# Linear attention by blocks of 64 tokens on quarter and half arrays, with scores and r stacked as one stationary operand

## The reference, cut to what matters

```
B, H, S, D = 4, 8, 768, 48
for t in range(S):
    cur = einsum('bhd,bhe->bhde', u * kt, vt)
    y[:, :, t] = einsum('bhd,bhde->bhe', rt, state + cur)
    state = w * state + einsum('bhd,bhe->bhde', kt, vt)
x = y as (3072, 384)
h = x @ w_in (384 x 2048);  g = max(h, 0) + alpha * min(h, 0);  x2 = g @ w_out (2048 x 384)
then 8 experts of 384 tokens each, chosen by the scores x2 @ w_gate
```

## Time and profile before

| | |
|---|---|
| median of 3 runs (lowest to highest) | 891.94 us (891.16 to 891.98) |
| the profiled execution | 890.23 us, span 888.5 us |
| PE busy | 832.6 us, 94% of the span |
| DVE, POOL, ACT busy | 461.7 us, 463.2 us, 212.3 us |
| chain that ended last | 82% of it on PE, 9% on DVE |

### The profile page before, as it was taken

The page is one execution under the profiler, slowest core; times in us unless marked ns, Lnnn a source line. Parts: engine busy times, 40 slices in busy tenths (PEclk is TensorE's granted clock), DMA queues, the critical chain, the costliest instruction groups (busy, mean ns, idle before and its releaser), DMA issues.

```text
span 888.5 us, 14960 instructions
## 1 busy us (share of the span) xinstructions
PE 832.6 (94%) x5562; PEld 723.7 (81%) x5562; DVE 461.7 (52%) x1005; ACT 212.3 (24%) x440; POOL 463.2 (52%) x448
## 2 busy tenths in 40 slices
PE   3989999999999999999999999955999999999996
PEld 2978887888788878887888888745888989989996
DVE  8554546444544464446444433367766767755221
ACT  1023312111211121112111221103142443333451
POOL 5669845443544444444444253206347757667872
PEclk9999999999999999999999999955999999999999
DMA  8454411111111111111000000014405405325410
GB/s 220 125 149 132 120 51 34 54 54 54 53 53 53 53 53 53 53 53 53 9 9 9 10 10 18 10 37 170 169 23 175 171 26 196 131 67 197 180 41 27
DMA packets 42788, 70.12 MB, mean 79 GB/s; under 512 B 5489, under 2 KB 28145, under 8 KB 42737
## 3 DMA queue, kind: packets, MB, share of 16 engines
q1 hardware_dynamic: 35632, 53.71, 18.6%
q0 software_dynamic: 3072, 9.44, 3.2%
q10 hardware_dynamic: 4032, 6.29, 2.5%
HBM read 59.99 MB, written 9.44 MB: 78 GB/s over the span
## 4 chain that ended last, share of the span: by engine, by line
PE 82%; DVE 9%; issue 4%; POOL 2%; ACT 1%; DMA 1%; POOLq 0%; SPq 0%; ACTq 0%; DVEq 0%
PE bank L981 22%; PE bank L983 20%; PE bank L982 20%; PE bank L1014 5%; PE bank L993 3%; PE bank L1025 3%; PE bank L1136 3%; PE bank L1010 2%; PE bank L1074 2%; DVE grid L879 1%; DVE grid L881 1%; PE bank L1037 1%; PE bank L1162 1%; PE bank L1152 1%; DVE xTl L667 1%
## 5 line engine op out<-in xcount | busy, mean ns | idle before, releaser
L384 POOL TENSOR_TENSOR gl<-g,gh 128x512 fp32r<-128x512 f32 x96 | 124.3, 1295 | 213.1 <-ACT gh L501 213.1
L716 DVE TENSOR_SCALAR q<-bank,alpha_sb 128x512 f32<-128x512 f32 x96 | 72.1, 751 | 173.8 <-PE bank L983 173.4
L501 ACT CAST gh<-g 128x512 fp32r<-128x512 f32 x96 | 59.6, 621 | 406.0 <-PE bank L983 363.0
L981 PE MATMUL bank<-gh,wout_h 128*128 128x512 f32 x288 | 120.3, 418 | 0.7 <-POOL gl L384 0.2
L981 PE MATMUL bank<-xTh,win_h 128*128 128x512 f32 x288 | 114.5, 398 | 5.6 <-DVE xTl L667 4.4
L983 PE MATMUL bank<-gh,wout_l 128*128 128x512 f32 x288 | 113.1, 393 | 0.0
L983 PE MATMUL bank<-xTh,win_l 128*128 128x512 f32 x288 | 112.7, 391 | 0.0
L982 PE MATMUL bank<-xTl,win_h 128*128 128x512 f32 x288 | 112.7, 391 | 0.0
L982 PE MATMUL bank<-gl,wout_h 128*128 128x512 f32 x288 | 112.4, 390 | 0.0
L436 POOL TENSOR_TENSOR w1l<-raw,w1h 128x384 fp32r<-128x384 f32 x64 | 66.3, 1036 | 60.3 <-ACT w2h L534 60.0
L981 PEld LDWEIGHTS bank<-xTh,win_h 128*128 128x128 f32 x288 | 54.4, 189 | 19.2 <-issue 6.1
(11 more groups left out here) (163 smaller groups left out, 1550.5 us busy)
## 6 DMA issues: line engine op xcount, KB each, us to landing
raw<-w SPq DMA_DIRECT2D x32, 768.0 KB, 5.7
kt<-kT SPq DMA_DIRECT2D x48, 96.0 KB, 2.5
rt<-rT SPq DMA_DIRECT2D x48, 96.0 KB, 2.6
kn<-kN SPq DMA_DIRECT2D x24, 192.0 KB, 2.8
rn<-rN SPq DMA_DIRECT2D x24, 192.0 KB, 2.9
vn<-v SPq DMA_DIRECT2D x24, 192.0 KB, 3.2
x2rows<-x2n SPq DMA_DIRECT2D x24, 192.0 KB, 1.9
x2T<-w_in ACTq DMA_DIRECT2D x12, 256.0 KB, 3.5
```

What stands on the lines that cost most here:

```text
L384: nc.gpsimd.tensor_tensor(gl[:, f % 2], g[:, f % 2], gh[:, f % 2].bitcast(F32), ALU.subtract).then_inc(gl_ready, 1)
L501: nc.scalar.copy(gh[:, f % 2], g[:, f % 2]).then_inc(gh_ready, 1)
L716: nc.vector.tensor_scalar(q[:, f % 2], h, 0.0, alpha_sb[:, f:f + 1], ALU.min, ALU.mult).then_inc(q_ready, 1)
L981: nc.tensor.matmul(o, a_h, b_h, start=first, stop=False)
```

## The change

A block keeps its 128 tokens, but is computed as two halves of 64 (j = 0, 1). For each half one stationary operand (`both`) holds the masked scores of 64 tokens in one half of the partitions and scaled r in the other, and one streamed operand (`vs`) holds the 64 rows of v and the state of 48 rows. `attend` is then 16 products of 128 rows and 64 stationary columns (in the first stage j = 0 has no state and takes 64 rows), `scores` 16 of 48 rows and 64 columns, `new_state` 16 of 64 rows and 48 columns. There are two states for each block, so `update` and `decay` come twice; `update` of half 0 now stands ahead of `attend`, and `new_state` ahead of `attend`. `scale` takes three instructions, k and r live in two buffers that are loaded after the scores two blocks before, v is loaded twice, and the loop over chunks is written out. In the first stage the order on PE and DVE is a new one. The diff, cut to its core (`attend`, `update` and the loops of before stand above):

```diff
+        def halves(j):
+            return slice(j * HALF, j * HALF + HALF)
+        def heads_in(j):
+            return slice((1 - j) * HALF, (1 - j) * HALF + D)
+        def y_bank(c):
+            return banks[0] if first(c) else banks[7]
+        def score_bank(c, b, j):
+            return banks[1 + j] if first(c) and b % 2 else banks[5 + j]
+        def state_bank(c, j):
+            return banks[3 + j] if first(c) else banks[5 + j]
+        def weights(c, b):
+            if not first(c) or b == 0:
+                return both
+            return (g[:], xT[:, 0:2], q[:])[b - 1].rearrange("p d (h t) -> p d h t", h=H)
...
             def load_rows(c, b):
-                for dst, src in ((kn, kN), (rn, rN), (vn, v)):
+                for dst, src in ((kn, kN), (rn, rN)):
                     sp.dma_start(dst[:, b], src[bass.ds(c, 1), :, b].rearrange("a t d -> (a t) d")).then_inc(rows_loaded[b], 16)
+                for j in range(2):
+                    sp.dma_start(vs[halves(j), b, j], v[bass.ds(c, 1), halves(j), b].rearrange("a t d -> (a t) d")).then_inc(v_loaded[b], 16)
+                sp.dma_start(vn[:, b], v[bass.ds(c, 1), :, b].rearrange("a t d -> (a t) d")).then_inc(v_loaded[b], 16)
 
...
+            def load_next_heads(c, b):
+                wait(sp, scores_done, 8 * c + 2 * b + 2)
+                sp.sem_inc(load_begun, 1)
+                if b + 2 < B:
+                    load_heads(c, b + 2)
+                else:
+                    load_heads(c + 1, b - 2)
...
             def decay(c, b):
 
-                pool.wait_ge(y_done, B * c + b + 1)
-                nc.gpsimd.tensor_tensor(state[:, b], state[:, b], cpow[:], ALU.mult).then_inc(s_decayed, 1)
+                pool.wait_ge(v_loaded[b], 48 * c + 48)
+                wait(pool, s_updated, 8 * c + 2 * b)
+                nc.gpsimd.tensor_tensor(decayed[:].rearrange("p (h d) -> p h d", h=H), vs[:, b, 0].rearrange("p (h d) -> p h d", h=H), cpow[:], ALU.mult).then_inc(s_decayed, 1)
+            def decay2(c, b):
+                pool.wait_ge(s_updated, 8 * c + 2 * b + 1)
+                nc.gpsimd.tensor_tensor(decayed[:].rearrange("p (h d) -> p h d", h=H), vs[:, b, 1].rearrange("p (h d) -> p h d", h=H), cpow[:], ALU.mult).then_inc(s_decayed2, 1)
...
                         if f % 4 == 0:
+                            decay(i + 1, b)
                             own(i + 1, b)
-                        if f % 4 == 1:
-                            decay(i + 1, b)
-                        if f % 4 == 2 and b + 1 < B:
-                            prepare(i + 1, b + 1)
+                        if f % 4 == 2:
+                            decay2(i + 1, b)
+                            if b + 1 < B:
+                                prepare(i + 1, b + 1)
...
+            pool.wait_ge(tables, 1)
+            prepare(0, 0)
             for b in range(B):
-                prepare(0, b)
+                if b + 1 < B:
+                    prepare(0, b + 1)
...
             def scale(c, b):
                 dve.wait_ge(heads_loaded[b], 64 * c + 64)
-                nc.vector.tensor_tensor(rt[:, b], rt[:, b], rpow[:], ALU.mult).then_inc(rk_scaled, 1)
-                nc.vector.tensor_tensor(kt[:, b], kt[:, b], kpow[:], ALU.mult).then_inc(rk_scaled, 1)
+                if not first(c):
+                    dve.wait_ge(y_done, B * c + b)
+                nc.vector.tensor_tensor(kt[:, b % 2], kt[:, b % 2], kpow[:], ALU.mult).then_inc(rk_scaled, 1)
+                for j in range(2):
+                    rows = halves(1 - j)
+                    nc.vector.tensor_tensor(weights(c, b)[rows, j], rt[rows, b % 2], rpow[rows], ALU.mult).then_inc(rk_scaled, 1)
 
...
             def mask(c, b):
...
+                for j in range(2):
+                    dve.wait_ge(scores_done, 8 * c + 2 * b + j + 1)
+                    rows = halves(j)
+                    nc.vector.tensor_tensor(weights(c, b)[rows, j], score_bank(c, b, j)[rows].rearrange("p (h t) -> p h t", h=H),
+                                            before[rows, rows].unsqueeze(1).to_broadcast([HALF, H, HT]), ALU.mult).then_inc(masked, 1)
 
...
+            def update(c, b, j):
+                to, of = heads_in(1 - j), heads_in(j)
+                if j == 0:
+                    dve.wait_ge(state_done, B * c + b + 1)
+                    if not first(c):
+                        dve.wait_ge(s_decayed, B * (c - 1) + b + 1)
+                    ins = nc.vector.tensor_copy(vs[to, b, 1], state_bank(c, j)[of, 0:DM]) if first(c) else nc.vector.tensor_tensor(
+                        vs[to, b, 1], state_bank(c, j)[of, 0:DM], decayed[of], ALU.add)
+                    ins.then_inc(s_updated, 1)
                     if first(c):
-                        ins = nc.vector.tensor_copy(state[rows, b, :, cols], new[rows, :, cols])
...
+                        nc.vector.tensor_tensor(decayed[to].rearrange("p (h d) -> p h d", h=H), state_bank(c, j)[of, 0:DM].rearrange("p (h d) -> p h d", h=H),
+                                                cpow[of], ALU.mult).then_inc(s_decayed2, 1)
+                else:
+                    if not first(c):
+                        dve.wait_ge(y_done, B * c + b + 1)
+                    dve.wait_ge(s_decayed2, B * c + b + 1)
+                    nc.vector.tensor_tensor(vs[to, b, 0], state_bank(c, j)[of, 0:DM], decayed[of], ALU.add).then_inc(s_updated, 1)
...
                         if f % 4 == 1:
+                            update(i + 1, b, 0)
+                        if f % 4 == 2:
                             attended(i + 1, b)
-                        if f % 4 == 2:
-                            update(i + 1, b)
-                        if f % 4 == 3 and b + 1 < B:
-                            scale(i + 1, b + 1)
-                            own(i + 1, b + 1)
+                        if f % 4 == 3:
+                            update(i + 1, b, 1)
+                            if b + 1 < B:
+                                scale(i + 1, b + 1)
+                                own(i + 1, b + 1)
...
             def scores(c, b):
-                pe.wait_ge(rk_scaled, 8 * c + 2 * b + 2)
-                wait(pe, masked, 8 * c + 2 * b - (2 if first(c) else 0))
+                pe.wait_ge(rk_scaled, 12 * c + 3 * b + 3)
+                if first(c):
+                    wait(pe, masked, 2 * b - 2)
+                else:
+                    pe.wait_ge(s_updated, 8 * c + 2 * b)
                 wait(pe, x2n_ready, B * (c - 2) + b + OUT_PRE)
                 wait(pe, logits_ready, B * (c - 2) + b + OUT_PRE)
...
+                for h in range(H):
+                    for j in range(2):
+                        mm = nc.tensor.matmul(score_bank(c, b, j)[halves(j), h * HT:(h + 1) * HT], kt[heads_in(j), b % 2, h], weights(c, b)[heads_in(j), j, h],
+                                              start=(h == 0), stop=(h == H - 1), skip_group_check=True)
+                        if h == H - 1:
                             mm.then_inc(scores_done, 1)
 
...
             def new_state(c, b):
+                pe.wait_ge(v_loaded[b], 48 * c + 48)
+                pe.wait_ge(kpad_ready, B * c + b + 1)
                 if first(c):
                     wait(pe, s_updated, 2 * b)
                 else:
-                    pe.wait_ge(x_ready, B * c + b + 1)
-                pe.wait_ge(kpad_ready, B * c + b + 1)
...
+                for h in range(H):
+                    cols = slice(h * D, (h + 1) * D)
+                    for j in range(2):
+                        mm = nc.tensor.matmul(state_bank(c, j)[heads_in(j), cols], kpad[halves(j), b % 2, cols], vs[halves(j), b, j, cols],
+                                              start=(h == 0), stop=(h == H - 1), skip_group_check=True)
                 mm.then_inc(state_done, 1)
+            def attend(c, b):
+                pe.wait_ge(s_updated, 8 * c + 2 * b + 1)
+                pe.wait_ge(masked, 8 * c + 2 * b + 2)
+                if first(c):
+                    wait(pe, x_ready, b)
+                elif isinstance(c, int) and c == 1 and b == 0:
+                    pe.wait_ge(first_l, B)
+                else:
+                    pe.wait_ge(xt_ready, B * (c - 1) + b)
+                for h in range(H):
+                    cols = slice(h * D, (h + 1) * D)
+                    for j in range(2):
+                        rows = halves(0) if first(c) and j == 0 else slice(0, P)
+                        mm = nc.tensor.matmul(y_bank(c)[halves(j), cols], weights(c, b)[rows, j, h], vs[rows, b, j, cols],
+                                              start=(h == 0), stop=(h == H - 1), skip_group_check=True)
+                mm.then_inc(y_done, 1)
...
-                        (scores, attend, new_state, turn)[f % 4](i + 1, f // 4)
+                        (scores, new_state, attend, turn)[f % 4](i + 1, f // 4)
...
-            for n in range(NPAIR):
-                mm = nc.tensor.transpose(banks[7][:, n * P:(n + 1) * P], down[:, n], ident)
```

(60 more changed lines are left out.)

140 lines of the change are left out of this document (49 added, 91 removed).

## The result

The changed kernel takes 907.4 us (median of 4 runs, 902.5 to 909.3) beside 891.95 for the kernel before: ratio 1.0167, with an interval from 1.0126 to 1.0208. It is 1.7% slower, where I had forecast 888 us. The profiled execution took 909.3, its span is 907.6 us.

The account below looks back on a forecast made before the run. PE was taken to bound the dense layer, busy 22.35 of 22.35 us per block. 890.2 - 24.0 + 14.2 + 3.5 + 2.0 = 885.9; the median lies 1.7 higher: 888 us, own range 880 to 896, overall 869 to 908.

Parts of the forecast that it names:

- attention parts shorter, 20 blocks: Dense layer: `scores`, `new_state` and `attend` together fall from 4.88 to 3.68 us per block, -24.0 us for 20.
- DVE late at steady block ends: Dense layer outside chunk 0: scalings end at 184.1, `scores` could start at 184.65; nothing late, so no cost.
- block ends of chunk 0, waits: POOL's weight work stretches DVE's scalings; PE waits 1.6, about the same and 0.3 us, +3.5 us.
- chunk starts: The third scaling ends about 0.4 us after `scores` had started before; five chunk starts, +2.0 us.
- first stage: Four blocks: `attend` +2.8 and `new_state` unchanged per block, plus 3 us for the new chain; +14.2 us.
- column halves run side by side: Dense-layer `attend`: members sharing rows but differing in columns run at once, 0.058 us a pair, 1.27 us in all.
- The alternation of 64 and 128 rows in the first stage: `attend` changes division at each of 16 products, 0.39 us each, so 6.2 us per block.
- its reading against the change: First stage: divisions differing in rows alone count as two modes and drain the array; +14.2 us, otherwise -2.2.
- The load of 64 columns: Dense-layer attention on the divided array: half of 0.107 plus the same 0.005, so 0.058 us.
- The step that failed: DVE at dense-layer block ends: `update` 0.50 us, then three scalings 0.60 apart; nothing late, by 0.5 us.
- rival 3: DVE late at every block end as POOL's `gl` doubles the last scaling; 0.7 us x 12, 896 us, chance 0.09.
- Rival 1: Column halves load one after the other; `attend` 1.79 + 0.34 us in the dense layer; 907 us, chance 0.30.

Follow-up runs that it names:

- e1: Changed kernel with the next block's three scalings one quarter of a block earlier; 898.1 us, ratio 0.9963 to the kernel before.
- e8: Changed kernel with one added wait: POOL's `gl` in a block's last quarter starts only after DVE's three scalings; 888.5 us, ratio 0.9962 to the kernel before.
- e5: e1 with dense-layer `attend` issuing all products of column half 0, then all of half 1; 900.9 us, ratio 1.0112 to the kernel before.
- e9: e4 with 64 rows for half 0 in dense-layer `attend`, alternating with 128, result altered; 936.8 us, ratio 1.0527 to the kernel before.
- e4: Changed kernel with the edits of e1 and e3, and a chunk's first scalings ahead of the preceding chunk's end; 871.2 us, ratio 0.9771 to the kernel before.
- e2: Changed kernel with first-stage `attend` issuing its eight 64-row products first, then its eight 128-row ones; 905.3 us, ratio 1.0028 to the kernel before.
- e3: Changed kernel with 128 rows in all first-stage `attend` products, half 0's update moved behind `attend`; 906.0 us, ratio 1.0051 to the kernel before.
- e7: Changed kernel without any edit, run on another chip; 906.5 us, ratio 1.0166 to the kernel before.

## Why the prediction was wrong

My sum against the rows, up to the mark (the kernel before 566.87, changed 584.62, +17.75):

| step | predicted | measured | from |
|---|---|---|---|
| attention parts shorter, 20 blocks | -24.0 | -26.0 | 22.35 - 21.05 (e1) = 1.30 each |
| DVE late at steady block ends | 0 | +10.9 | 12 x (21.96 - 21.05) |
| block ends of chunk 0, waits | +3.5 | +6.3 | 2.02 + 2.15 + 2.12 |
| the lower clock behind them | none | about +4.7 | windows under e8 |
| chunk starts | +2.0 | +4.8 | 4 waits of 1.2 (e1) |
| first stage | +14.2 | +16.6 | 55.51 to 72.11, first `scores` of chunk 1 |
| sum | -4.3 | +17.3 | |

**What held.** The blocks' saving, with its parts. `scores` takes 1.07 us from its start at 275.73 to the next product at 276.80, and with 0.11 behind and 0.08 ahead (the distances to the dense neighbours beyond 0.23) 1.26, where I had 1.27; `new_state`, from 281.12 to 281.98 and the same edges, 1.04 instead of 1.14; `attend` is 1.07 in e1 without its edges, about 1.25 with them, instead of 1.27. That column halves run side by side, which no row of before showed, is e5's 0.73 us. The alternation of 64 and 128 rows in the first stage: 6.10 us for 6.2 predicted. The Trainium skill's rule ("TensorEngine Tiling (Array Packing)", Key Properties) that a change of tiling mode drains the engine came out as its reading against the change had it: divisions that differ in rows alone count as two modes (3.90 us against 1.07 at the full clock, 6.10 against 1.95 in the first stage; e9, e4). The load of 64 columns, set at 0.058 us from a split of 0.112 into 0.107 and 0.005 that no row shows, came to 1.81 us / 32 = 0.057 in e5. The loop written out and the DMAs cost nothing.

**The step that failed** is "At the end of a block DVE has `update` of half 1 ... Nothing is late, by 0.5 us." Behind it stood 0.60 us from start to start for all three scalings. In the trace the last is late by 0.85, 1.35 us away from my number: 1.0 because it collides with `gl`, the rest because the starts lie 0.58 to 0.73 apart and not 0.50 to 0.60. My rival 3 named this mechanism ("since POOL's `gl` of 1.3 us begins at 183.5 and can double the last scaling"), at 0.7 us and 12 places, 896 us, and I gave it 0.09. The row that spoke for it was already among mine: in chunk 0, where POOL is always busy, the same scalings took 1.35 and 1.50 us instead of 0.68. I took 1.35 us for chunk 0 and 0.68 elsewhere. In the sum `gl`'s start at 183.5 never stands beside the third scaling that I myself let end at 184.1; it stands in the rival alone. This step by itself is worth 10.9 us and turns 888, faster, into 899, slower than before; the other 9 are the sizes below, the clock and the first stage.

**The sizes that were off.** In chunk 0 I let DVE be late by 1.6, 1.6 and 0.3 us; it was 2.0 to 2.15 each time. That the third block end would be better had no row behind it. At the chunk starts (0.4 for 1.2) the two `both` take 2.11 us, as at a block end, here beside POOL's `kpad` (253.62, 1.46 us) and `decayed` (255.05, 1.46 us), which I had not laid beside them either. In chunk 0 the cause is in part that of the failed step: e8, which moves `gl` alone, takes the waits from 6.3 to 3.7 us. At the chunk starts e8 changes nothing, as `gl` doesn't stand there. That `kpad` and `decayed` are the cause there is an argument from the rows, which no run tests; e4 shows only that the waits go when the scalings stand elsewhere.

**What I had not thought of** was the granted clock in the dense layer. I had tied it to the first stage only. Two of the changed kernel's three waits of some 2 us were followed by 1.2 GHz. The other traces agree: in the dense layer of e1, e2, e3, e4 and e7 seven of eight waits of PE, of 1.84 to 2.33 us, were followed by such a stretch, and in e3, e7 and e8 none of five from 1.26 to 1.76. So I take the waits for the cause of these 4.7 us, but that is argued and not shown: two waits, of 2.02 and 1.96 us, were followed by none, and in e9 the clock fell seven times behind an `attend` of alternating products, without any wait. What decides stays open.

Rival 1 had the right number, 907 us, and the wrong mechanism. Only the blocks' inside tells them apart: it had `attend` at 2.1 us and no waits, the trace has 1.1 and 0.85 of waiting.

## What to carry to other kernels

When a change adds an instruction to an engine whose slack is below a microsecond, lay every instruction of the engine that can slow it beside the new end, at its own start time, and price the collision with the longest row of the same instruction, not with the shortest. If the slack is gone, look first at what could be moved for nothing: here one quarter of a block earlier, or one wait on the other engine, was worth 18 us.

On a divided array, keep neighbours in the same division: filling up the rows with zeros was cheaper (1.95 us for `attend` in the first stage) than leaving them out (6.10).

## What the runs showed of the hardware

- A product of 64 rows next to one of 128 rows costs about 0.24 us at the full clock and 0.38 in the first stage, against 0.07 and 0.12 where neighbours agree (3.90 and 6.10 against 1.07 and 1.95 us for 16).
- A DVE instruction with two inputs in the on-chip memory stretched from 0.69 to 1.67 us beside POOL's, and POOL's from 1.27 to 1.50.
- Two column halves of the array on the same 128 rows take their loads side by side (1.14 us for 32 records, 1.87 one by one).
- The granted clock in the rows need not tell the level of the first stage. In the changed kernel and the one before it reads 1.00 in the whole first stage, also where the same records last 1.52 us that later last 0.92. In e5 it reads 0.50 from 44 us on, and `attend`, whose program is the same there, takes the same 6.10 us:

```profile
44.00:65.00 21.00, 18.49 (x143) 13.96 (x142) 8.17 (x16) 1.90 (x5) 4.67 (x5) 0.50 0.42 132
```
```profile
47.95 6.10 PE L1085 MATMUL bank<-vs,xT 64*64 64x48 f32 x32 [0.74 <-DVE vs L698]
```

  By these equal durations the first stage of the changed kernel ran at the lower level of 1.2 GHz too, as the prediction took it from durations alone. In e3 some of its records take 0.92 us in the middle of that stage, so its clock isn't fixed either.
